# All outputs of an attention unit behind the three output blocks of an expert's chunk

## What is computed

```python
scores = scale * np.matmul(q, k.transpose(0, 1, 3, 2))
mask = (rel >= 0) & (rel < window)
scores = np.where(mask, scores, -1000000000.0)
attn = np.exp(scores - np.max(scores, axis=-1, keepdims=True))
attn = attn / (np.sum(attn, axis=-1, keepdims=True) + 1e-09)
x = np.matmul(attn, v)                       # tokens x 512
for e in range(E):                           # E = 4
    out += p[:, e:e+1] * (np.maximum(x @ w1[e], 0.0) @ w2[e])
h = out @ w_in
result = (h * np.cos(h)) @ w_out
```

## Time and profile before

| | before |
|---|---|
| median of 3 timed runs | 637.68 us (636.98 to 638.14) |
| the profiled execution | 638.28 us |
| its span | 636.3 us |
| PE busy | 630.0 us (99%) |
| DVE, ACT, POOL busy | 301.6, 261.0, 272.1 us |
| mean granted clock of PE | 0.999 |

### The profile page before, as it was taken

The page is one execution under the profiler, slowest core; times in us unless marked ns, Lnnn a source line. Parts: engine busy times, 40 slices in busy tenths (PEclk is TensorE's granted clock), DMA queues, the critical chain, the costliest instruction groups (busy, mean ns, idle before and its releaser), DMA issues.

```text
span 636.3 us, 10157 instructions
## 1 busy us (share of the span) xinstructions
PE 630.0 (99%) x3652; PEld 564.2 (89%) x3652; DVE 301.6 (47%) x726; ACT 261.0 (41%) x558; POOL 272.1 (43%) x405
## 2 busy tenths in 40 slices
PE   8999999999999999999999999999999999999997
PEld 7887899989999999999998888998999999999996
DVE  5754431215433415433315433426775667766564
ACT  5885322223321223321223321246655468544542
POOL 5893246697720296720296720287000069400000
PEclk9999999999999999999999999999999999999999
DMA  9775000012220012210022220033100012001011
GB/s 288 246 238 173 38 1 1 1 66 67 67 66 1 1 66 66 66 66 0 1 66 67 67 66 1 11 122 100 34 0 1 2 37 97 1 0 49 0 51 50
DMA packets 23432, 37.25 MB, mean 59 GB/s; under 512 B 2784, under 2 KB 16096, under 8 KB 23392
## 3 DMA queue, kind: packets, MB, share of 16 engines
q1 hardware_dynamic: 23104, 36.33, 18.2%
q10 hardware_dynamic: 288, 0.39, 0.2%
HBM read 34.36 MB, written 2.36 MB: 58 GB/s over the span
## 4 chain that ended last, share of the span: by engine, by line
PE 98%; DVE 1%; DMA 1%; issue 0%; ACT 0%; DVEq 0%
PE bank L1285 31%; PE bank L1312 31%; PE bank L1343 16%; PE bank L1329 14%; PE bank L1227 2%; PE bank L1263 2%; PE bank L1252 1%; PE bank L1429 1%; DMA k_t<-in_k 1%; DVE acc L1070 0%; PE bank L1473 0%; DVE s_sb L890 0%; ACT prob L618 0%; DVE prob_t L939 0%; DVE prob_t L921 0%
## 5 line engine op out<-in xcount | busy, mean ns | idle before, releaser
L466 POOL TENSOR_TENSOR w_lo<-w_raw,w_hi 128x128 fp32r<-128x128 f32 (+1 forms) x244 | 144.9, 629 | 212.7 <-ACT w_hi L670 211.2
L1285 PE MATMUL bank<-x_hi,w_hi 128*128 128x384 f32 (+1 forms) x384 | 131.2, 342 | 0.0
L1285 PE MATMUL bank<-x_hi,w_lo 128*128 128x384 f32 (+1 forms) x384 | 129.1, 336 | 0.0
L1285 PE MATMUL bank<-x_lo,w_hi 128*128 128x384 f32 (+1 forms) x384 | 128.8, 335 | 0.0
L1312 PE MATMUL bank<-w_hi,hp_hi 128*128 128x512 f32 x288 | 114.5, 398 | 0.1
L1312 PE MATMUL bank<-w_hi,hp_lo 128*128 128x512 f32 x288 | 113.6, 394 | 0.0
L1312 PE MATMUL bank<-w_lo,hp_hi 128*128 128x512 f32 x288 | 112.1, 389 | 0.0
L1023 DVE TENSOR_TENSOR h_raw<-bank,h_raw 128x384 f32<-128x384 f32 x84 | 46.7, 556 | 91.8 <-PE bank L1329 91.8
L1285 PEld LDWEIGHTS bank<-x_hi,w_hi 128*128 128x128 f32 x384 | 72.2, 188 | 2.9 <-issue 0.5
L1285 PEld LDWEIGHTS bank<-x_lo,w_hi 128*128 128x128 f32 x384 | 72.2, 188 | 1.5
L954 DVE SCALAR_TENSOR_TENSOR hp_lo<-bank,hp_hi 128x384 fp32r<-128x384 f32 x48 | 26.5, 556 | 98.1 <-ACT hp_hi L702 57.2
(11 more groups left out here) (112 smaller groups left out, 972.5 us busy)
## 6 DMA issues: line engine op xcount, KB each, us to landing
w_raw<-in_weights SPq DMA_DIRECT2D x43, 512.0 KB, 3.6
q_t<-in_q SPq DMA_DIRECT2D x12, 192.0 KB, 5.4
result<-acc SPq DMA_DIRECT2D x9, 256.0 KB, 2.1
w_raw<-in_weights SPq DMA_DIRECT2D x8, 256.0 KB, 6.0
k_t<-in_k SPq DMA_DIRECT2D x8, 224.0 KB, 5.6
v_w<-in_v SPq DMA_DIRECT2D x4, 384.0 KB, 5.0
v_w<-in_v SPq DMA_DIRECT2D x4, 320.0 KB, 5.9
v_w<-in_v SPq DMA_DIRECT2D x4, 192.0 KB, 4.3
```

The source lines that it names most:

```text
L466: last = nc.gpsimd.tensor_tensor(w_lo[:, f, at:at + part], raw[:, at - begin:at - begin + part], w_hi[:, f, at:at + part], ALU.subtract)
L1285: last = nc.tensor.matmul(ps[:, 0:TOK], w[:, f, chunk(c)], x[:, c, token_cols(t)], start=c == 0 and i == 0, stop=c == DC - 1 and i == 2)
```

## The change

In the first turn, for every chunk but f = 4, all nine output products of the chunk now come first, then the outputs of the unit, then the scores of unit m + 3. Before, one output block came ahead of the outputs and two after them. Since block 1 and 2 are now written at once, the wait for three split chunks (`hp_lo_done` of OC = 3) stands ahead of all nine products of chunk 0. For f = 4 the order stays.

DVE in the first turn: `copy_first(9)` moves from chunk 5 to between the two halves of the maxima of unit 11, in chunk 4.

In the opening, WARM grows from 5 to 7. ACT takes the first exponential of unit 1's second head ahead of `x_high_part` of unit 0, with a semaphore of its own (`piece_maxed`), the other two after it. DVE takes `masked_maxima(1, 0)` before `invert_part(1)`, and puts `copy_second_early(1)` behind the first of the three maxima of `masked_maxima(2, 1)` instead of behind all three.

```diff
-WARM = 5
+WARM = 7
@@ ACT
             exponentials(1, 0)
             high_channels(0)
+            act.wait_ge(piece_maxed, 1)
+            exponential(3, 0)
             for t in range(CT):
                 x_high_part(t)
-            exponentials(1, 1)
+            act.wait_ge(maxed, head_count(1, 1))
+            exponential(3, 1)
+            exponential(3, 2).then_inc(exped, 1)
@@ DVE
             invert_part(0)
-            invert_part(1)
             dve.wait_ge(masks, ALL_MASKS)
             masked_maxima(1, 0)
+            invert_part(1)
             invert_part(2)
@@
-            masked_maxima(2, 1)
+            masked_maxima(2, 1, (0,))
             copy_second_early(1)
+            masked_maxima(2, 1, (1, 2))
@@
-                    if f != FIRST:
+                    if f not in (FIRST, FIRST + 1):
                         copy_first(m)
@@
                     masked_maxima(m + SCORED, 0)
+                    if f == FIRST:
+                        copy_first(m + 1)
                     masked_maxima(m + SCORED, 1)
@@ PE
-                down_cells(f, (0,), -1)
-                if f == FIRST:
-                    down_cells(f, (1,), -1)
+                if f != FIRST:
+                    if f == 0:
+                        pe.wait_ge(hp_lo_done, OC)
+                    down_cells(f, range(OC), -1).then_inc(down_done, 1)
+                    outputs(m)
+                    if m + SCORED < UNITS:
+                        scores(m + SCORED)
+                else:
+                    down_cells(f, (0, 1), -1)
                     scores(m + SCORED)
                     transpose_probs(m, 1)
                     down_cells(f, (2,), -1).then_inc(down_done, 1)
                     outputs(m)
-                else:
-                    outputs(m)
-                    if f == 0:
-                        pe.wait_ge(hp_lo_done, OC)
-                    down_cells(f, (1, 2), -1).then_inc(down_done, 1)
-                if m + SCORED < UNITS and f != FIRST:
-                    scores(m + SCORED)
```

More of the change, by code:

```diff
@@ L222, in build @@
         maxed = sem("maxed")
+        piece_maxed = sem("piece_maxed")
         exped = sem("exped")
@@ L908, in masked_maxima @@
                     last = masked_maximum(m, h, t)
+                    if (m, h, t) == (1, 1, 0):
+                        last.then_inc(piece_maxed, 1)
                 if CT - 1 in ts:
```

## The result

| | before | after |
|---|---|---|
| median of 6 timed runs, alternating | 637.90 us (636.98 to 638.28) | 640.53 us (640.34 to 640.96) |
| ratio, 95% interval | | 1.0051 (1.0041 to 1.0061) |
| the profiled execution, its span | 638.28, 636.3 us | 640.34, 638.5 us |

The change makes the kernel slower by 2.6 us by the medians, 3.3 us by the ratio (2.6 to 3.9). Forecast were +2.3 us and 640.0, range 637.8 to 641.3. The time lies in the range; the step of +2.3 us is smaller than both readings of the measured one.

A forecast was written before the change was run, and what follows sets the result against it. PE's own instruction list was taken to bound the kernel (98% of the chain). First turn +2.0, opening +0.56 and zeros -0.3 gave +2.3 us on a median of 637.68: 640.0 us, range 637.8 to 641.3.

The forecast's parts named there:

- first up product to chunk 0's output products due: Opening: two maxima wait for DVE's copy, exponentials and x_lo come later, PE's up products of unit 1 start 0.56 us later.
- chunk 3, to unit 8's transposes: Chunk 3: transposes opening chunk 4 wait for x_lo, +0.51 us; changeover saving less a 0.15 wait gives -0.10.
- chunks 4 and 5, to unit 10's transposes: Unit 9's copy behind three maxima instead of six saves 0.32 us; chunk 5's transposes waiting for x_lo cost 0.10.
- The mechanism: First turn and opening: PE waits for values that now come late, x_lo and hp_lo, without slack; waits sum to 2.0 + 0.56 us.
- The 0.1 us of chunks 5 and 6: Chunks 5 and 6: from first output product to next transposes 4.43 instead of 4.33 us, +0.10 us each.
- Chunk 0: PE waits 0.76 us for the third split before its output products and saves 0.20 of changeovers: +0.56 us.
- Chunk 7: Next turn's first up product waits for unit 11's x_lo with nothing between: 4.43 instead of 3.26 us, +1.17.
- The zeros: Opening: two more zero products may raise PE's clock early; bounds -1.2 and +0.1 us, taken at -0.3.
- a sign of being wrong: Transposes of 273 ns in the first 9 us, chunks of 6.76 us, or no idle row at the turn's end.
- first rival: Opening: the clock rises early in most runs, giving back 1.2 us while all waits stay: +1.4, 639.1 us; chance 0.21.
- Chunks 1 to 3: Second transposes wait for DVE's first copy, 0.26, 0.26 and 0.15 us, against 0.25 saved per chunk: 0, 0, -0.10.

The follow-up runs named there:

- a2: Kernel before with only PE's new order (all nine output products, outputs, scores): ratio 1.0052, +2.9 us from the first up product on.
- b1: Changed kernel with PE's old order in chunk 7 alone: ratio 1.0032 to before, -1.3 us against the changed kernel.
- a3: Kernel before with only the wait for three split chunks moved ahead of chunk 0's first output block: ratio 1.0018, +0.9 us.
- b4: Changed kernel with DVE's first copy ahead of the hidden split in chunks 1 to 3: ratio 1.0039 to before, -1.0 us against the changed kernel.
- a4: Kernel before with only copy_second_early(1) put behind the first of three maxima of unit 2's second head: ratio 1.0016, +0.4 us.
- c1: Changed kernel with all three maxima of unit 2's second head ahead of copy_second_early(1) again: ratio 1.0045 to before, -0.6 us against the changed kernel.
- b2: Changed kernel with DVE's four small share operations of chunk 6 moved ahead of x_low(10): ratio 1.0047 to before, -0.4 us against the changed kernel.
- a1: Kernel before with WARM = 7 (seven zero products) and nothing else: ratio 0.9998, median 637.27 us against 637.21.
- c3: Kernel before with WARM = 1 (one zero product) and nothing else: ratio 1.0002, median 637.59 us against 637.21.
- b5: Kernel before with outputs and scores side by side, output blocks behind them, in chunks 0 to 3, plus unit 9's earlier copy: 635.86 us against 637.26, ratio 0.9977.

## Why the prediction was right, and where its sizes were off

Starts on PE in the two profiled executions, from place to place. PE is due at chunk 0's output products in the kernel after at 33.09 + 0.18 = 33.27, where the last up product ends its turn:

| stretch | before | after | moved | predicted |
|---|---|---|---|---|
| first up product to chunk 0's output products due | 12.74 to 33.73 | 11.72 to 33.27 | +0.56 | +0.56 |
| chunk 0, to the next up product | to 37.76 | to 38.04 | +0.74 | +0.56 |
| chunks 1 and 2 | to 51.78 | to 52.10 | +0.04 | 0 |
| chunk 3, to unit 8's transposes | to 58.80 | to 59.54 | +0.42 | +0.41 |
| chunks 4 and 5, to unit 10's transposes | to 71.21 | to 71.71 | -0.24 | -0.22 |
| chunk 6, to unit 11's transposes | to 77.20 | to 77.81 | +0.11 | +0.10 |
| chunk 7, to the next turn's first up product | to 82.09 | to 84.17 | +1.47 | +1.17 |

- **The mechanism** held in every place of the table: a2 carries most of the loss, b1 takes 1.3 of it back, a3 shows the wait of chunk 0 by itself, b4 the one in chunks 1 to 3, a4 and c1 the one in the opening. The 0.1 us of chunks 5 and 6 stands in the rows alone; no experiment takes it by itself.
- **Chunk 0** was 0.18 short: PE waited 34.12 - 33.27 = 0.85 instead of 0.76, and the first product after a wait takes 0.31 to the next start instead of 0.23.
- **Chunk 7** was 0.30 short. I followed x_lo to the next up product, but not to the copy behind it on DVE; b2 shows that term (0.4).
- **The zeros** were the term without a basis: taken at -0.3 for the median, near 0 in a1 and c3, whose interval of 0.6 us either way does not exclude it. The sum put it in by choice between its bounds, with the slow opening of one profiled run as the usual one. What the prediction named as a sign of being wrong, transposes of 273 ns in the first 9 us, nearly came: 294 ns in the kernel after. The condition of its first rival, an early clock, thus held in that profiled run, whose first up product came 12.74 - 11.72 = 1.02 us earlier, not the full 1.2, with 0.7 us of waiting for POOL in it. The rival's 639.1 us did not come, since the runs of before seem to have had the faster opening mostly, as four of the seven profiled runs with five products had.
- **Chunks 1 to 3**: the wait was right, the saving that it ate was too small (0.33 instead of 0.25).

With 0 for the zeros and the two missing terms (0.18, 0.30) the sum is 3.1 us, against 3.2 in the profiles. That the forecast of 640.0 lies only 0.5 us below the measured 640.53 is in part luck: the first three runs of before had a median of 637.68, the 27 runs beside a1 to a4 one of 637.21, and a larger step from a lower start ends at nearly the same time. What moves the opening's pace from run to run with five products stays open.

## What to carry to other kernels

Putting a product of the bounding engine ahead of the work that others wait for takes its cover away: measure the chain behind that work (here 2.18 us from outputs to the next use of the bank), and leave at least as much of the engine's own work behind it. Follow the chain to each instruction queued behind its end, not only to the one that waits for it. An order that saves changeovers and keeps the cover can exist: b5, which leaves one or two blocks behind outputs and scores in chunks 0 to 3 and the old order in chunks 5 to 7, is 1.4 us faster than before where the order of the change cost 2.9.

## What the runs showed of the hardware

A changeover between products of different shape costs PE 0.09 to 0.11 us each way (output product to outputs to output product), 0.33 us a chunk with the wait that stood in it. PE's opening pace differed from run to run: the transposes up to 9 us took 421 ns in before, a3 and c3, and 294 in after, while the granted clock of these stretches reads 1.00 in all four. Two runs with seven products differed too: the first scores took 400 ns in a1 and 277 in after.
